# Attention, two MLP layers and a Fourier transform on one core: the order of a DMA queue, two fold sums, and the opening

## What is computed

```python
def _attn_ref(q, k, v, alpha):                      # a linear recurrence per head
    for t in range(S):
        state = alpha[:, :, t, :, None] * state + np.einsum('bhd,bhe->bhde', k[:, :, t], v[:, :, t])
        y[:, :, t] = np.einsum('bhd,bhde->bhe', q[:, :, t], state)

def _moe_ref(x, g_ln, w_ch1, w_ch2):                # first layer, on the heads side by side
    xn = (x - mu) / np.sqrt(var + 1e-06) * g_ln
    return x + np.maximum(xn @ w_ch1, 0.0) @ w_ch2

def _moe2_ref(x, w_ch1, w_ch2):                     # second layer
    u = x + np.real(fft(fft(x, axis=1), axis=2))
    un = (u - mu) / np.sqrt(var + 1e-06)
    return u + np.maximum(un @ w_ch1, 0.0) @ w_ch2
```

## Time and profile before

| | |
|---|---|
| median of 3 runs | 755.38 us |
| the profiled execution | 755.05 us |
| its span, first to last instruction | 752.9 us |
| mean granted TensorE clock | 0.998 |
| TensorE busy | 737.0 us (98%) |
| VectorE busy | 457.1 us (61%) |
| ScalarE busy | 338.1 us (45%) |
| GpSimd busy | 57.0 us (8%) |

### The profile page before, as it was taken

One profiled execution on the slowest core, in us unless ns is written; L12 is line 12 of the kernel. 1 busy time (PEld: TensorE's weight loads), 2 busy tenths in 40 slices (PEclk: granted clock), 3 DMA queues, 4 the chain that ended last, 5 costly groups with the idle time before them and its releaser, 6 DMA issues.

```text
span 752.9 us, 16980 instructions
## 1 busy us (share of the span) xinstructions
PE 737.0 (98%) x6898; PEld 709.7 (94%) x6898; DVE 457.1 (61%) x1072; ACT 338.1 (45%) x562; POOL 57.0 (8%) x112
## 2 busy tenths in 40 slices
PE   8999999999999999999899999999999999999998
PEld 7989999889999888899899999999999999999998
DVE  7988877857578576685686764347444664343322
ACT  3443233656666566566543344143422434141511
POOL 1100000000000000000005000300021000200000
PEclk9999999999999999999999999999999999999999
DMA  9362223383552835746343422040103101010200
GB/s 257 109 170 78 69 83 95 79 192 87 134 135 69 191 81 110 153 122 153 86 140 119 160 63 55 2 136 33 32 33 116 52 12 51 0 33 31 38 27 31
DMA packets 91730, 68.07 MB, mean 90 GB/s; under 512 B 58709, under 2 KB 86601, under 8 KB 91657
## 3 DMA queue, kind: packets, MB, share of 16 engines
q1 hardware_dynamic: 91656, 67.06, 34.4%
HBM read 43.65 MB, written 13.37 MB: 76 GB/s over the span
## 4 chain that ended last, share of the span: by engine, by line
PE 77%; DVE 9%; DMA 7%; ACT 4%; issue 2%; SPq 1%; DVEq 0%; ACTq 0%
PE h L119 12%; PE acc L119 11%; PE h L121 11%; PE h L120 11%; PE acc L121 11%; PE acc L120 11%; DMA kT_planes<-k_planes 2%; DMA a_in<-alpha_dram 2%; DVE F_inv L1213 2%; PE side_bank L120 2%; PE side_bank L121 2%; PE side_bank L119 2%; DVE F L1200 1%; DMA q_in<-q_dram 1%; PE side_bank L1722 1%
## 5 line engine op out<-in xcount | busy, mean ns | idle before, releaser
L188 ACT ACTIVATE hT_high<-h 128x384 fp32r<-128x384 f32 (+1 forms) x204 | 96.0, 471 | 263.3 <-PE h L121 262.9
L119 PE MATMUL h<-xnT_high,w_high 128*128 128x384 f32 (+1 forms) x612 | 206.5, 337 | 4.9 <-DVE hT_low L193 3.8
L193 DVE SCALAR_TENSOR_TENSOR hT_low<-h,hT_high 128x384 fp32r<-128x384 f32 (+1 forms) x204 | 108.2, 531 | 163.9 <-ACT hT_high L188 163.4
L121 PE MATMUL h<-xnT_high,w_low 128*128 128x384 f32 (+1 forms) x612 | 199.3, 326 | 0.0
L120 PE MATMUL h<-xnT_low,w_high 128*128 128x384 f32 (+1 forms) x612 | 199.1, 325 | 0.0
L119 PE MATMUL acc<-w_high,hT_high 128*128 128x384 f32 x576 | 195.8, 340 | 2.4 <-DVE hT_low L193 2.3
L121 PE MATMUL acc<-w_high,hT_low 128*128 128x384 f32 x576 | 193.4, 336 | 0.0
L120 PE MATMUL acc<-w_low,hT_high 128*128 128x384 f32 x576 | 193.1, 335 | 0.0
L119 PEld LDWEIGHTS h<-xnT_high,w_high 128*128 128x128 f32 x612 | 115.2, 188 | 10.6 <-DVE hT_low L193 5.7
L120 PEld LDWEIGHTS h<-xnT_low,w_high 128*128 128x128 f32 x612 | 115.4, 189 | 0.0
L121 PEld LDWEIGHTS h<-xnT_high,w_low 128*128 128x128 f32 x612 | 115.1, 188 | 0.0
(11 more groups left out here) (160 smaller groups left out, 823.5 us busy)
## 6 DMA issues: line engine op xcount, KB each, us to landing
stage<-w_dram SPq DMA_DIRECT2D x24, 384.0 KB, 3.5
x_scratch<-x_unit SPq DMA_DIRECT2D x8, 576.0 KB, 3.5
a_in<-alpha_dram SPq DMA_DIRECT2D x6, 672.0 KB, 5.2
q_in<-q_dram SPq DMA_DIRECT2D x6, 672.0 KB, 7.6
k_in<-k_dram SPq DMA_DIRECT2D x6, 672.0 KB, 9.6
v_in<-v_dram SPq DMA_DIRECT2D x6, 576.0 KB, 3.9
xb<-x_scratch SPq DMA_DIRECT2D x4, 576.0 KB, 4.5
xb<-x_turned SPq DMA_DIRECT2D x4, 576.0 KB, 7.3
```

Source lines behind the costliest of these rows:

```text
L119: pe.matmul(out, wh, xh, start=start, stop=False)
L121: return pe.matmul(out, wl, xh, start=False, stop=stop)
L188: act.activation(self.hT[0][:, j % H_SLOTS, 0:u.cols], self.hps[j % H_BANKS][:, 0:u.cols], ACT.Relu).then_inc(self.h_high, 1)
L193: dve.scalar_tensor_tensor(out=self.hT[1][:, j % H_SLOTS, 0:u.cols], in0=self.hps[j % H_BANKS][:, 0:u.cols], scalar=0.0, in1=self.hT[0][:, ...
```

## The change

- SP: for each unit, `load_a(u)` comes first. The copies that stood between the turns of y and k now stand behind `turn_k(u, 0)` and ahead of `store_x1`.
- VectorE: for the first batch `fold_rows` moves from slot 10 to slot 9; `fold_turned_rows` stands in slot 10 ahead of `high_front`.
- GpSimd clamps the chunks 1, 2 and 3 of the first batch in place of VectorE: two before `final_rows(ONE[0])`, one behind it. Chunk 4, on VectorE, waits for them.
- The second chunk's k in `ONE[0]` is transposed into `m.acc[2]`; the wait on `u_read` moves from the transposes to the increments.
- The outputs of `ONE[0]` signal after each of their two halves (`first_y`, `y_summed`), and ScalarE copies each half for itself.
- ScalarE splits weight piece 2 ahead of the second `copy_y`; VectorE splits piece 1 behind the second centring.

```diff
--- before.py
+++ after.py
@@ -424,6 +424,7 @@
         y_begun = sem("y_begun")
+        first_y = sem("first_y")
         y_summed = sem("y_summed")
@@ -503,6 +504,9 @@
 
+        def kT_bank(u, c):
+            return m.acc[2] if u.first() and c == 1 else bank[BKU]
+
         def first_y_bank(two):
@@ -638,18 +642,16 @@
 
-            AFTER_Y = {5: (0, 0), 6: (0, 2), 7: (1, 0), 8: (1, 2)}
+            AFTER_X = {5: (0, 0), 6: (0, 2), 7: (1, 0), 8: (1, 2)}
             AFTER_STORE = {5: (0, 1), 7: (1, 1)}
...
                 attending = ONE[u.n - 1]
+                load_a(u)
                 if attending in REGULAR:
...
                     turn_y(attending, 0)
-                    x1_stored(AFTER_Y[u.n][0] + 1)
-                    turn_rows(*AFTER_Y[u.n])
                     turn_k(attending, 2)
                     turn_y(attending, 1)
-                load_a(u)
                 load_q(u)
@@ -658,6 +660,9 @@
                 turn_k(u, 0)
+                if u.n in AFTER_X:
+                    x1_stored(AFTER_X[u.n][0] + 1)
+                    turn_rows(*AFTER_X[u.n])
                 store_x1(u.b - 1, u.c0 // UT)
@@ -840,7 +845,18 @@
 
+            def bound_chunk(g):
+                pool.wait_ge(first_a[g], 16)
+                pool.wait_ge(a_bounded, g)
+                if g >= UT:
+                    pool.wait_ge(F_inv_ready, g - UT + 1)
+                pool.tensor_scalar(a_safe[:, g % UT, :], a_in[:, g % UT, :], A_LOW, A_HIGH,
+                                   ALU.max, ALU.min).then_inc(a_bounded, 1)
+
+            bound_chunk(1)
+            bound_chunk(2)
             final_rows(ONE[0])
+            bound_chunk(3)
             for i in range(ONE[0].size):
@@ -901,7 +917,7 @@
                 act.wait_ge(kT_summed, u.base + c + 1)
-                act.activation(k_divT[:, :, :], bank[BKU][:, 0:PAIRS * R].rearrange("p (h k) -> p h k", h=PAIRS),
+                act.activation(k_divT[:, :, :], kT_bank(u, c)[:, 0:PAIRS * R].rearrange("p (h k) -> p h k", h=PAIRS),
                                ACT.Copy).then_inc(kT_copied, 1)
@@ -944,13 +960,15 @@
             def copy_y(u, c):
-                act.wait_ge(y_summed, u.base + c + 1)
+                if not u.first():
+                    act.wait_ge(y_summed, u.base + c + 1)
                 if c == 0 or u.slot(c) == 0:
...
                     for two in range(2):
+                        act.wait_ge((first_y, y_summed)[two], c + 1)
                         op = act.activation(odd_even(to)[:, two, :, :], of_pairs(first_y_bank(two)[:, 0:PAIRS * D]),
@@ -1077,8 +1095,8 @@
             split.high(act, ONE_W[1])
+            split.high(act, ONE_W[2])
             copy_y(ONE[0], 1)
-            split.high(act, ONE_W[2])
             act.wait_ge(g_loaded, 16)
@@ -1181,6 +1199,7 @@
                 if g >= UT:
+                    dve.wait_ge(a_bounded, g)
                     dve.wait_ge(F_inv_ready, g - UT + 1)
@@ -1431,6 +1450,8 @@
                 if slot == 10:
+                    if not following:
+                        fold_turned_rows(0, 0)
                     for k in range(KD):
@@ -1535,7 +1556,6 @@
             prepare_k(ONE[0], 0)
-            bound_chunk(1)
             prepare_q(ONE[0], 1)
@@ -1547,10 +1567,9 @@
             centre(ONE[0], (0,))
-            split.low(dve, ONE_W[1])
             final_statistics(ONE[0], (1,))
             centre(ONE[0], (1,))
-            bound_chunk(2)
+            split.low(dve, ONE_W[1])
             for i in range(ONE[0].size):
@@ -1573,7 +1592,6 @@
                     prepare_k(u, 0)
-                    bound_chunk(3)
                 if j == 4:
@@ -1625,9 +1643,8 @@
                     split.low(dve, TABLES[j - 5])
-                if j == 10:
+                if j == 9:
                     fold_rows(0, 0)
-                    fold_turned_rows(0, 0)
             fold_cols(0, 0)
@@ -1697,12 +1714,14 @@
                 pe.wait_ge(k_ready, u.base + c + 1)
-                if c > 0:
+                if u.first():
+                    pass
+                elif c > 0:
                     pe.wait_ge(u_read, u.base + c)
-                elif not u.first():
+                else:
                     pe.wait_ge(m.xnT_ready, KD * u.n)
                 for h in range(PAIRS):
-                    op = pe.transpose(bank[BKU][:, h * R:(h + 1) * R], k_div[:, u.slot(c), h, :], ident[0:R, 0:R])
+                    op = pe.transpose(kT_bank(u, c)[:, h * R:(h + 1) * R], k_div[:, u.slot(c), h, :], ident[0:R, 0:R])
                 op.then_inc(kT_summed, 1)
@@ -1749,6 +1768,8 @@
                 wait_v(ONE[0], c)
+                if c > 0:
+                    pe.wait_ge(u_read, c)
                 for h in range(PAIRS):
@@ -1770,7 +1791,7 @@
                                        start=c == h == 0, stop=h == PAIRS - 1)
-                op.then_inc(y_summed, 1)
+                    op.then_inc((first_y, y_summed)[two], 1)
```

## The result

The kernel after takes 743.25 us (median of 6 runs, 742.79 to 744.83), the one before 755.27 us beside it (6 runs, 752.48 to 756.54): a ratio of 0.9847 [0.9828, 0.9866]. The sign, the places and most sizes held; the gain from alpha was 6.2 us where I took 3.8, and the cost of new waits on k was smaller than I took it.

What follows compares the result with a forecast made beforehand. TensorE, busy 737.0 of 752.9 us, was taken as the bound, with its idle time in the first 375 us to be won. 755.38 - 5.8 (alpha, k) - 3.8 (fold) + 1.4 (new waits) + 0 (opening) = 747.2 us; range 744.9 to 750.3.

Steps and rivals of the forecast that it cites:

- Alpha first: Regular units: alpha's load issued earlier in SP's queue ends TensorE's five low-half waits, 3.8 us gained.
- k's waits: TensorE's waits on k near 156.9 and 250.6 go with the copies behind the turns: 2.0 us gained.
- New waits on the second k: Units 5 and 7: copies, store and alpha delay the second k's turn; 0 to 2.8 us lost, 1.4 taken.
- Fold: Near 370 us: fold sums moved earlier end a 2.28 us wait and 1.5 us of half clock, 3.8 us gained.
- Opening: Up to 25 us: the edits together give between 0.5 us gained and 2.8 us lost; 0 taken.
- the port rival: Opening: GpSimd's clamps hold VectorE's port, clamps 1 and 2 costing 0.5 to 1.6 us each: 748.2 to 750.0, chance 0.10.
- Nothing is late: Rival: the turns are not held and TensorE has no new gap: 745.8 us, chance 0.22.
- The queue's cost: Rival: second k's new waits cost all 2.8 us, plus up to 2 for y's planes: 748.6 to 750.5, chance 0.16.
- the late alpha: Rival: VectorE's own work in slots 6 to 8 is late, four 0.8 us waits stay: 750 us, chance 0.03.
- the slower end: Rival: units 5 and 7, second k so late that TensorE's clock falls, not faster: 758.4 us if 3.3 later, chance 0.05.

Runs made afterwards that it cites:

- e5: Kernel before with only alpha's load moved ahead of the turn of k, copies in their old place: 751.41 us, ratio 0.9926.
- e1: Kernel before with only SP's queue changed, alpha's load first and copies behind the turns: 748.69 us, ratio 0.9901.
- e9: Kernel after with VectorE clamping alpha twice in units 4 to 8: 745.88 us, ratio 0.9878.
- e10: Kernel after with VectorE clamping alpha three times in units 4 to 8: 751.77 us, ratio 0.9952.
- e6: Kernel before with only the copies moved behind the turns, alpha's load in its old place: 754.70 us, ratio 0.9980.
- e11: Kernel after with the second parts of the copies moved from units 5 and 7 to units 6 and 8: 742.57 us, ratio 0.9829.
- e3: Kernel before with only all the opening edits: 755.67 us, ratio 0.9996.
- e2: Kernel before with only the two fold sums moved earlier: 751.17 us, ratio 0.9940.
- e4: Kernel before with the queue and fold edits, without the opening's: 743.65 us, ratio 0.9829.
- e7: Kernel after with the clamps of chunks 1 to 3 back on VectorE: 743.90 us, ratio 0.9831.
- e12: Kernel after with second copies moved to units 6 and 8, clamps back on VectorE, weight splits in the old order: 742.45 us, ratio 0.9822.

## Why the prediction was wrong, step by step

**Alpha first: the mechanism right, its size wrong, and this is the step that failed.** "I take all 3.8 us" read the total of the waits in the earlier trace rows as the gain. The starts moved by 6.2 us. The sum can be made from the trace that I had. Each of the five shown waits costs its idle time, and 0.16 us more because the matmul that waited would have started under the one before it (0.33 lasted less 0.17 between starts), and 0.11 us more because the next one comes 0.28 us behind it: 3.8 + 5 x 0.27 = 5.2 us, where the starts show 5.0. And in slot 11 of each unit, and once more in the first, VectorE was late by so little that TensorE shows no bracket: five places at 172.9, 177.9, 224.7, 273.6 and 322.1, 0.25 to 0.32 us each, 1.5 us together. That is 6.5 us by the starts, of which 0.3 stay in after. e5 takes the same places away by alpha's move alone, e1 shows it with k's part (7.6 us), and e9 and e10 show that VectorE's lateness brings such losses back. With 6.2 in place of 3.8 us the sum comes to 744.8 us, and with k, the new waits and the fold as measured below to 743.9; the 0.7 us from there to 743.25 are inside the interval of the measured ratio and go to no term.

**k's waits: right.** 2.0 us forecast, 2.2 measured at the two places. e6's profiled execution adds what I did not ask: with k's wait gone, more of alpha's lateness reaches TensorE.

**New waits on the second k: too dear.** I counted all on the few engines that the copies hold and took the middle of 0 and 2.8 us, 1.4. Measured are 0.44 us of idle at unit 7 (0.48 by the starts), none at unit 5, and 0.23 at 341.4 (0.30 by the starts), on the third k of unit 8, where I had counted nothing and whose cause is open: 0.8 us in all. SP's order of time in after, and ScalarE's, show unit 5's case:

```profile
181.74 0.72 SPq L628 DMA_DIRECT2D x_turned<-x_scratch  x1
185.28 2.47 SPq L565 DMA_DIRECT2D a_in<-alpha_dram  x1
189.00 1.29 SPq L580 DMA_TRANSPOSE kT_planes<-k_planes  x1
```

```profile
193.60 1.23 ACT L915 ACTIVATE k_divT<-kT_planes 128x896 uint16<-128x896 uint16 x1 [3.27 <-DMA kT_planes<-k_planes]
```

SP itself is held for 2.47 us at alpha's issue, which I had said would not happen. The turn is in by 193.6 where my count, moved by the 0.6 us that all stands earlier here, gave 195.6: the count is wrong by 2 us. Alpha needs 7.5 us from its issue and lands at 192.8, where the count gave 193.5; the turn follows 0.8 us behind, where I had put 2.1. So most of the error is the last step, and a strict order of store, copy, alpha and turn isn't refuted by these times. The Trainium skill (DMA: Bandwidth & Descriptors, the section on queues, rings and completion order) has a ring of its own for each queue and engine, so that a transfer's share on other engines need not wait for a copy; whether that happened here no row tells. The copies do hold alpha and the turn a little: in e11, with the second copy moved away, alpha lands in 4.9 us and no wait is left.

**Fold: right in sum, its second half by luck.** 3.8 us forecast, 3.9 by the starts (2.44 and 1.64 less 0.16). VectorE had the room in slot 9 and in the wait for the join that I read there, and nothing was late next. But that the half clock belongs to this wait, 1.5 us of the sum, isn't shown: full clock followed waits of 2.3 us (e1) and 3.1 us (e3) at the fold and one of 1.7 us on k (e2); half clock came with 2.3 us at the fold (before), followed 1.7 us (e3) and 2.2 us (e5) on k, came with 3.0 us at the fold (e5, e6), and came in the dummy matmuls of the opening (after, e1, e4, e7). What the move does change is how often such a stretch appears. Executions with a mean clock of 1.000 were 3 of 24, 2 of 17 and 2 of 17 of the kernel before; 6 of 37 with the wait at the fold left in (e1, e3, e5, e6) and 43 of 62 with it gone (after, e2, e4, e7 to e12). By the mean clocks, an estimate: what they fall short of 1.000, times 755 us, is 2.4 us in an execution before and in those with the wait left, and 0.5 us with it gone. So as a mean the 1.5 us are about right: 1.9 us by this estimate.

**Opening: right as far as the runs can tell, 0 forecast, and e3 measured 0.9996.** Its parts differ from what I had. GpSimd's clamp takes four times what the memset row gave (GpSimd's order of time in after):

```profile
8.02 2.19 POOL L853 TENSOR_SCALAR a_safe<-a_in 112x512 f32<-112x512 f32 x1 [3.88 <-DMA a_in<-alpha_dram]
15.91 2.07 POOL L853 TENSOR_SCALAR a_safe<-a_in 112x512 f32<-112x512 f32 x1 [5.70 <-DMA a_in<-alpha_dram]
...
20.07 1.92 POOL L853 TENSOR_SCALAR a_safe<-a_in 112x512 f32<-112x512 f32 x1 [1.65 <-DMA a_in<-alpha_dram]
```

Both my ends, 0.5 and 1.6 us, lie below it. VectorE's scan waits for it, 0.8 us in after, e9 and e11 and 0.27 in e3 and 0.28 in e10. In e3 the own bank and the halves give that back; in e9, e10 and e11, 0.4 us later than before at the first hidden matmul, they do not. The first hidden matmul was at 26.47 in after, past the 25.5 that I had set as the mark of the port rival; but that execution ran at a clock of 0.66 from 20 to 25, which no port explains, and at full clock e3 had 24.82 and the other three 25.3 to 25.4, short of the mark.

**The rivals.** "Nothing is late" is nearest (waits of 0.9 us in place of 0), and its price, 745.8, fails by the same mis-sized term: with 6.2 for 3.8 it is 743.4. The queue's cost, the late alpha and the slower end are refuted by the waits above. The port: VectorE did not stand for the length of GpSimd's clamp. In its order of time its operation with two inputs in SBUF runs inside the clamp's 8.02 to 10.21, at 0.85 us in place of 0.69; in four other executions beside the clamp it took 0.69 to 0.98. The wait of 0.80 us behind it is for the clamp's result:

```profile
8.59 0.85 DVE L1255 TENSOR_TENSOR k_div<-k_in,F_inv 112x512 f32<-112x512 f32 x1
10.24 1.37 DVE L1219 TENSOR_TENSOR_SCAN F<-a_safe,zeros 112x128 f32<-112x128 f32 x4 [0.80 <-POOL a_safe L853]
```

The range failed on one side because I bounded the unseen costs only; the gain that stood in a row had no bounds at all.

## What to carry to other kernels

The idle time in a table of waits is a lower bound of what a wait costs where instructions overlap: measure a stretch by the starts of the same instructions, and look for starts wider apart than the usual step with no idle beside them. Look at two late inputs together, since one can hide the other: in e6 the end of k's wait at 156.9 won 1.66 us, and 2.4 us of waits behind alpha came out after it. Give a range to the gains that the profile shows, not only to the costs that it doesn't.

## What was unexpected of the hardware

- A late TensorE matmul of 384 columns cost 0.27 us beyond the idle time shown, by the starts, and one just late some 0.3 us with none shown.
- The stretch of half clock behind 370 in before cost 1.6 us by the starts. Such a stretch came at 21, 158 or 366 to 373 us, and the length of the wait before didn't foretell it: 1.7 us was followed by half clock in e3 and by full clock in e2.
- GpSimd's clamp of 512 float32 elements in each of 112 partitions took 1.91 to 2.46 us over all profiles; VectorE's operations beside it ran on, at most 0.29 us slower (0.98 in place of 0.69 in e9).
